# Attention steps regrouped into one TensorE visit per layer step, and the split of g moved forward, in a fused attention and feed-forward kernel

## The reference

```
q_d, k_d, v_d = means over 4 neighbouring tokens of q, k, v        # B=4, H=8, S=576, D=64
out_up    = repeat(softmax(q_d k_d^T / 8) v_d, 4)                   # coarse attention, 144 x 144
out_local = softmax(mask(q k^T / 8, |i-j| < 4)) v                   # banded attention
x = (out_up + out_local) as [2304 tokens, 512]
x = max(0.01 h, h) @ w_out    with h = x @ w_in                     # layer 1, d_ff = 2048
x = (h - tanh(h)) @ w_out2    with h = x @ w_in2                    # layer 2
```

## Time and profile before

| | |
|---|---|
| median of 3 runs | 996.45 us (994.6 to 997.91) |
| profiled execution, its own time | 992.21 us |
| span of the profiled execution | 990.4 us |
| outside the span | 1.8 us |
| PE busy | 955.1 us, 96% |
| weight load on PE busy | 891.5 us, 90% |
| DVE, ACT, POOL busy | 583.2, 554.5, 410.9 us (59%, 56%, 41%) |
| mean granted TensorE clock | 0.991 |
| layer 1, from its first hidden group to its last down group | about 67.8 to 580.4 us |

### The profile page before, as it was taken

How to read it: one execution, slowest core, us unless ns; L and a number is a source line. 1 busy time by engine, 2 the same in 40 slices (tenths; PEclk the granted TensorE clock), 3 DMA queues, 4 the chain that set the end, 5 groups by cost and what they waited for, 6 DMA issues and landing times.

```text
span 990.4 us, 19687 instructions
## 1 busy us (share of the span) xinstructions
PE 955.1 (96%) x6960; PEld 891.5 (90%) x6960; DVE 583.2 (59%) x1066; ACT 554.5 (56%) x1355; POOL 410.9 (41%) x341
## 2 busy tenths in 40 slices
PE   6788999999999999999999999999999999999998
PEld 5678999999999999999999999889899899898996
DVE  5556653663555546536324867876676676766764
ACT  3445544544645536445354767775575666766654
POOL 3446631823625517327071747633233233233232
PEclk9979999999999999999999999999999999999999
DMA  5762421122012201210200302100000000000000
GB/s 125 163 180 64 129 50 26 25 49 49 23 26 49 49 22 26 49 27 1 65 1 23 117 13 85 43 34 0 1 32 1 32 0 0 32 0 0 32 1 32
DMA packets 87222, 41.48 MB, mean 42 GB/s; under 512 B 59777, under 2 KB 80769, under 8 KB 87169
## 3 DMA queue, kind: packets, MB, share of 16 engines
q1 hardware_dynamic: 87168, 40.78, 15.4%
HBM read 36.04 MB, written 4.72 MB: 41 GB/s over the span
## 4 chain that ended last, share of the span: by engine, by line
PE 76%; POOL 6%; ACT 6%; DVE 5%; issue 3%; DMA 2%; SPq 2%; ACTq 0%; POOLq 0%; DVEq 0%
PE ph L473 11%; PE ph L475 11%; PE ph L474 11%; PE acc L549 6%; PE acc L550 6%; PE acc L551 6%; PE acc L502 6%; PE acc L503 5%; PE acc L504 5%; PE banks L371 2%; PE banks L403 2%; DVE g_lo L871 2%; POOL pl L992 2%; PE banks L390 2%; POOL g_lo L1038 1%
## 5 line engine op out<-in xcount | busy, mean ns | idle before, releaser
L1038 POOL TENSOR_TENSOR g_lo<-scratch,g_hi 128x384 fp32r<-128x384 f32 x96 | 125.6, 1309 | 257.7 <-ACT g_hi L663 257.7
L886 DVE TENSOR_TENSOR g<-g,ph 128x288 f32<-128x288 f32 x128 | 57.9, 453 | 187.7 <-ACT g L683 186.8
L1008 POOL TENSOR_TENSOR in_lo<-w_whole,in_hi 128x512 fp32r<-128x512 f32 x64 | 84.0, 1312 | 160.8 <-ACT in_hi L647 159.4
L473 PE MATMUL ph<-x_hi,w_hi_a 128*128 128x288 f32 (+1 forms) x448 | 144.5, 322 | 1.9 <-DVE x_lo L866 1.9
L475 PE MATMUL ph<-x_hi,w_lo_a 128*128 128x288 f32 (+1 forms) x448 | 140.4, 313 | 0.0
L474 PE MATMUL ph<-x_lo,w_hi_a 128*128 128x288 f32 (+1 forms) x448 | 140.3, 313 | 0.0
L683 ACT ACTIVATE g<-ph 128x288 f32<-128x288 f32 x128 | 52.5, 410 | 155.9 <-PE ph L475 154.4
L922 DVE SCALAR_TENSOR_TENSOR scratch<-scratch,ph 128x384 f32<-128x384 f32 x96 | 53.2, 554 | 108.4 <-ACT scratch L728 103.8
L1013 POOL TENSOR_TENSOR out_lo<-w_whole,out_hi 128x512 fp32r<-128x512 f32 x64 | 86.5, 1351 | 56.2 <-ACT out_hi L651 55.6
L727 ACT ACTIVATE scratch<-ph 128x384 f32<-128x384 f32 x96 | 46.8, 488 | 108.4 <-PE ph L475 106.8
L871 DVE TENSOR_TENSOR g_lo<-g,g_hi 128x288 fp32r<-128x288 f32 x128 | 90.5, 707 | 2.7 <-ACT g_hi L663 2.7
(11 more groups left out here) (162 smaller groups left out, 2689.9 us busy)
## 6 DMA issues: line engine op xcount, KB each, us to landing
out_dram<-o_stage SPq DMA_DIRECT2D x18, 256.0 KB, 2.0
w_whole<-in_moe_w_in_dram SPq DMA_DIRECT2D x16, 256.0 KB, 4.2
w_whole<-in_moe_w_out_dram SPq DMA_DIRECT2D x16, 256.0 KB, 4.3
qn<-in_q_dram SPq DMA_DIRECT2D x28, 144.0 KB
kn<-in_k_dram SPq DMA_DIRECT2D x28, 144.0 KB
v4n<-in_v_dram SPq DMA_DIRECT2D x28, 144.0 KB
vw<-in_v_dram SPq DMA_DIRECT2D x28, 122.5 KB
scratch<-in_moe_w_in_dram SPq DMA_DIRECT2D x8, 256.0 KB, 2.7
```

The lines of the kernel that those rows point to most:

```text
L473: pe.matmul(bank, whi, x_hi[:, c, 0:width], start=(c == 0), stop=False)
L1008: pool.tensor_tensor(in_lo[:, f % 2, :], w_whole[:, f - KEPT, 0:DM], in_hi[:, f % 2, :].bitcast(F32), ALU.subtract).then_inc(in_lo_done, 1)
L1038: pool.tensor_tensor(g2_lo[:, f % 3, :], g2[:, f % 2, :], g2_hi[:, f % 3, :].bitcast(F32), ALU.subtract).then_inc(g_lo_done, 1)
```

## The change

The 17 attention steps of a later pair are cut into 8 groups, one per step f of layer 1, and 16 groups (two pairs) fill the 16 steps of a mixed tile. A group's PE part is issued as one visit, behind the down group. Steps (8, 9, 10) have no PE part. The first two groups of the next pair stand in the last two steps of a tile, as steps 0 to 3 did before.

The chain leak, max, rounding, rest is now done for step f within step f on ACT and DVE, ahead of their attention steps; before, rounding and rest of step f-1 came behind leak and max of step f. The max writes back into the PSUM tile `ph1`, the rounding and the rest read it there, and H(f+2), which overwrites it, waits for the rest (`g_lo_done`) and no longer for the max. `split_in` stands ahead of the rounding, `split_out` of step f at the end of step f on ACT and POOL; before, it was at the start of step f+1 (for the last one behind `next_x` on ACT).

```diff
+GROUPS = ((0, 1), (2, 3), (4, 5), (6, 7), (8, 9, 10), (11, 12), (13, 14), (15, 16))
+GROUP_HEAD = 2
-        def later(slot, tile):
-            return (slot + HEAD) % STEPS, A, 2 * tile + 2 + (slot + HEAD) // STEPS
+        def later(f, tile, last):
+            if f < last:
+                pair, group = divmod(f + GROUP_HEAD, len(GROUPS))
+                for step in GROUPS[group]:
+                    yield step, A, 2 * tile + 2 + pair
...
 # PE
-                wait_from(pe, g_done, n - 1)
+                wait_from(pe, g_lo_done, n - 1)
...
                     if f < CF and not (begun and f == 0):
                         hidden1(tile, f)
-                    between(2 * f)
                     if ahead and f == CF + LAG1 - 1:
                         hidden1(tile + 1, 0)
                     if f >= LAG1:
                         down1(tile, f - LAG1)
-                    between(2 * f + 1)
+                    for step, s, i in later(f, tile, last):
+                        attention(step, s, i)
...
 # ACT
-                    if f - 1 >= KEPT:
-                        split_out(tile, f - 1)
                     if f < CF:
                         act.wait_ge(h_done, n + 1)
-                        wait_from(act, g_lo_done, n - 1)
+                        wait_from(act, g_done, n - 1)
                         act.activation(g1[:, f % 2, :], ph1[:, f % 2, 0:T1], ACT.Copy, scale=0.01)\
                             .then_inc(leak_done, 1)
                     if f == 0:
                         keep_before()
-                    if f:
-                        split_g(n - 1, f - 1, g1[:, (f - 1) % 2, :], g1_hi)
-                    between(2 * f)
                     if KEPT <= f + 2 < CF:
                         split_in(tile, f + 2)
+                    if f < CF:
+                        split_g(n, f, ph1[:, f % 2, 0:T1], g1_hi)
+                    for step, s, i in later(f, tile, last):
+                        attention(step, s, i)
                     extra(f)
-                    between(2 * f + 1)
+                    if KEPT <= f < CF:
+                        split_out(tile, f)
...
 # DVE
-                dve.tensor_tensor(g1_lo[:, f % 3, :], g1[:, f % 2, :], g1_hi[:, f % 3, :].bitcast(F32),
+                dve.tensor_tensor(g1_lo[:, f % 3, :], ph1[:, f % 2, 0:T1], g1_hi[:, f % 3, :].bitcast(F32),
...
-                        dve.tensor_tensor(g1[:, f % 2, :], g1[:, f % 2, :], ph1[:, f % 2, 0:T1], ALU.max)\
+                        dve.tensor_tensor(ph1[:, f % 2, 0:T1], g1[:, f % 2, :], ph1[:, f % 2, 0:T1], ALU.max)\
                             .then_inc(g_done, 1)
                     if f == 0:
                         keep_before()
-                    if f:
-                        lo_of_g1(n - 1, f - 1)
-                    between(2 * f)
+                    if f < CF:
+                        lo_of_g1(n, f)
+                    for step, s, i in later(f, tile, last):
+                        attention(step, s, i, (i + 2) // CD, (i + 2) % CD)
                     extra(f)
-                    between(2 * f + 1)
...
 # POOL
-                    if f - 1 >= KEPT:
-                        split_out(tile, f - 1)
-                    between(2 * f)
                     if KEPT <= f + 2 < CF:
                         split_in(tile, f + 2)
-                    between(2 * f + 1)
+                    for step, s, i in later(f, tile, last):
+                        attention(step, s, i)
+                    if KEPT <= f:
+                        split_out(tile, f)
```

More of the change, by code:

```diff
@@ L505, in down1, with layer1 @@
                 last.then_inc(y_done, 1)
-            def layer1(tile, between, begun=True, ahead=True):
+            def layer1(tile, last, begun=True, ahead=True):
                 for f in range(CF + LAG1):
@@ L561, in layer2 @@
                         down2(tile, f - LAG2)
[L563 to L570, removed]
             pe.wait_ge(const_ready, 1)
@@ L576, in _ @@
             pe.wait_ge(B.bank_free[1], uses1(2, 0))
-            mixed(0, begun=False)
+            layer1(0, CF, begun=False)
             with pe.Fori(1, MIXED - 1) as tile:
-                mixed(tile)
-            mixed(MIXED - 1, 2 * STEPS - HEAD)
+                layer1(tile, CF)
+            layer1(MIXED - 1, CF - GROUP_HEAD)
             for tile in range(MIXED, TILES1):
-                layer1(tile, nothing, ahead=tile < TILES1 - 1)
+                layer1(tile, 0, ahead=tile < TILES1 - 1)
             layer2(0, begun=False)
@@ L669, in keep_y, with layer1 @@
                         .then_inc(y_kept_act, 1)
-            def layer1(tile, between, extra, keep_before, ahead):
+            def layer1(tile, last, extra, keep_before, ahead):
                 for f in range(CF + 1):
@@ L698, in next_x, with mixed @@
                 split_x(x1_hi, T1, tile, CF * tile)
[L700 to L704, removed]
+            def mixed(tile, keep_before, last=CF):
+                layer1(tile, last, nothing, keep_before, lambda: next_x(tile + 1))
             def nothing(f=None):
@@ L779, in _ @@
                 mixed(tile, lambda: keep_y(tile - 1))
-            mixed(MIXED - 1, lambda: keep_y(MIXED - 2), 2 * STEPS - HEAD)
+            mixed(MIXED - 1, lambda: keep_y(MIXED - 2), CF - GROUP_HEAD)
             for tile in range(MIXED, TILES1):
                 last = tile == TILES1 - 1
-                layer1(tile, nothing, w2a if last else nothing, lambda: keep_y(tile - 1),
+                layer1(tile, 0, w2a if last else nothing, lambda: keep_y(tile - 1),
                        nothing if last else lambda: next_x(tile + 1))
@@ L1014, in split_out, with layer1 @@
                                    ALU.subtract).then_inc(out_lo_done, 1)
-            def layer1(tile, between):
-                for f in range(CF + 1):
+            def layer1(tile, last):
+                for f in range(CF):
                     if isinstance(tile, int) and tile == 0 and EARLY <= f + 2 < KEPT:
                         split_kept(f + 2)
-                    if f - 1 >= KEPT:
-                        split_out(tile, f - 1)
-                    between(2 * f)
                     if KEPT <= f + 2 < CF:
                         split_in(tile, f + 2)
-                    between(2 * f + 1)
[L1027 to L1034, removed]
+                    for step, s, i in later(f, tile, last):
+                        attention(step, s, i)
+                    if KEPT <= f:
+                        split_out(tile, f)
             def lo_of_g2(tile, f):
@@ L1077, in _ @@
                 attention(step, s, i)
-            mixed(0)
+            layer1(0, CF)
             with pool.Fori(1, MIXED - 1) as tile:
-                mixed(tile)
-            mixed(MIXED - 1, 2 * STEPS - HEAD)
+                layer1(tile, CF)
+            layer1(MIXED - 1, CF - GROUP_HEAD)
             with pool.Fori(MIXED, TILES1) as tile:
-                layer1(tile, nothing)
+                layer1(tile, 0)
             for f in range(CF):
```

## The result

The changed kernel takes 1013.37 us (median of 4 runs, 1012.1 to 1014.97), the kernel before 996.7 us (4 runs): ratio 1.0175, 95% interval 1.0158 to 1.0191. I had forecast 1004 us with a range up to 1011. The direction was right, and the size was less than half of what came. The profiled execution took 1015.0 us, its span is 1013.2 us.

A forecast was written before the change was run, and what follows sets the result against it. PE, busy 96% of the span, was taken to bound the kernel; the terms summed to +7.7 us on the profiled 992.2 us, and the same sum on the median of 996.45 gave 1004 us, range 997 to 1011.

The forecast's parts named there:

- The bound and the places: PE's order of work sets the time; in mixed tiles it stops at the turn and the ahead-run hidden group.
- The first pair's chain: Softmax chain of a tile's first pair: waiting for the same step's rounding twice delays the turn 1.2 us, +6.1 us total.
- The rest in PSUM: On DVE, the rest reading PSUM escapes POOL's hold: mean near 0.45 us, no stop for `g_lo`.
- The first `x_lo`: At a mixed tile's start, POOL's `out_lo` holds it: a 1.45 us stop in place of 0.46, +5.0 us for five.
- The first tile: PE's 2.59 us wait for the rest, held by POOL's weight split, goes; with joined visits -1.5 us.
- The second pair: In each tile's second pair, a chain of 11.0 us and a stop of 0.6 in place of 0.4, +1.2 us for six.
- rival C: POOL's queue in the second pair decides, DVE is held and D(10) waits for `out_lo`: another 7.8 us, 1012 us; chance 0.10.
- rival A: At tile starts `x_lo` slips ahead of `out_lo` or ACT finishes sooner; the seven starts cost nothing: 997.4 us; chance 0.10.
- rival B: Softmax chain less stiff, row maximum starting before 214.4; neither pairs nor starts stall: -8.7 us, 988 us; chance 0.12.
- The start of a tile: `out_lo` on POOL holds the first `x_lo`: +5.0 us for five mixed starts, +1.8 us for two plain ones.
- The joined visits: Attention visits on PE joined, fewer returns to large matmuls: 0.36 us saved a pair, -3.9 us total.
- The plain starts: At the two plain tiles' starts, `out_lo` holds `x_lo` and PE waits: +0.9 us each, +1.8 us total.

The follow-up runs named there:

- e3: Changed kernel with the grouping alone: leak, max, rounding and rest as before the change, g in SBUF; 1017.34 us, ratio 1.022.
- e4: Kernel before with the forward chain alone: rounding and rest of a step in that step, max and rest in PSUM; 1001.79 us, ratio 1.006.
- e5: Changed kernel with VectorE's row maximum and row sum ahead of the rest of the same step; 998.95 us, ratio 1.003.
- e2: Changed kernel with POOL's three sums of v of a tile's first pair moved behind that pair's normalizations; 1002.68 us, ratio 1.0073.
- e6: Changed kernel with the last step's out_hi behind x_hi on ScalarE, and row maximum and row sum ahead of the rest on VectorE; 985.59 us, ratio 0.9898.
- e1: Changed kernel with the last step's out_hi behind the next tile's four x_hi on ScalarE, as before the change; 997.84 us, ratio 1.002.

## Why the forecast fell short

**Right.** The bound and the places: PE stops at the turn and at a tile's start, and nowhere else in the mixed tiles. The first pair's chain: 1.2 forecast, 1.14 measured, undone by e3, made alone by e4, and taken away by e5. The rest in PSUM is free of POOL: 458 ns on average where it was 667. The first `x_lo` is held by `out_lo`: a stop of 1.45 forecast, 1.40 measured. The first tile: -1.5 and -1.9. The second pair: a chain of 11.0 us forecast, 10.95 measured (250.48 to 261.43), and a stop of 0.6 forecast, 0.55 measured. No queue on POOL decides there (rival C); what I had not seen is that this pair's subtraction on DVE lay under `out_lo` before (1.83 us) and is free of it now (0.82 us), since `out_lo` stands later. Nothing slipped in ahead of `out_lo` (rival A), and rival B's condition did not hold: the row maximum started 3.6 us after the scores ended, where it was 3.1.

**The step that failed** is "The start of a tile". It says that POOL starts `out_lo`, that this holds the first `x_lo`, and goes on as if POOL were idle after it. The three sums of v of the next pair, which stand right behind that `out_lo` in POOL's queue, have no term and no sentence in it. They could be seen in the trace of the kernel before, whose `out_lo` ended at 207.23:

```profile
207.40 0.74 POOL L985 TENSOR_TENSOR vd<-v4n 72x256 f32<-72x256 f32 x1 [0.17 <-DMA vw<-in_v_dram]
```

There the four `x_lo` were long done (204.51 to 206.07). Now the three sums alternate with the other `x_lo`: 1.5 us a start, 7.5 us (shown by e2). They also made a pattern of short stops behind a long one, behind which TensorE ran at half clock at three starts: 4.4 us, in no term and no rival of mine. Both together are 11.9 us; the two sums in the table lie 11.6 apart, and the forecast and the median 9.4.

**Mis-sized terms.** The joined visits saved about 0.9 us a tile, not 0.7, nearly all of it behind the products with v. The plain starts cost 1.36 us each, not 0.9; 0.25 of that is a late H(2), whose PSUM tile now waits for the rest behind `keep_y`. In layer 2 one more down group waits for POOL than before (0.95 us), where POOL splits that layer's weights (a stop that e4 has too and e3 has not, so it comes with the forward chain; why, no run shows), and the little won at the end of layer 1 is given back.

**Open**: why the clock falls at three starts of the changed kernel and at one of e5, with the same stops. What PE does between the starts does not tell them apart: in e5 the tiles ahead of all of the last four starts take 68.22 to 68.23 us with the same stops, and only the last one falls; in the changed kernel the tiles ahead of the second start (it holds) and the third (it falls) take 70.34 and 70.35 us. The moment at which the stops come may count. No run here moves it alone.

## What to carry to other kernels

When an instruction moves, write down the whole queue of the engine behind it and let each entry start as early as its own waits allow: what follows at once may now meet work of another engine that was long done before. When a producer is made earlier by waiting on another engine in the middle of a queue, put the work that the critical chain needs ahead of that wait. Here that was worth 12.3 us (e6 against e1); with `out_hi` behind `x_hi` as well, a loss of 1.7% became a gain of 1.0%, and with the next tile's x further ahead one of 1.3%. And a stop of PE is to be priced with what the clock may do behind it.

## What the hardware showed

A VectorE instruction with two SBUF inputs and a GpSimd instruction that reads SBUF alternated strictly, one for one, four times in a row: 3.89 us for the four VectorE instructions, which take 1.56 us where GpSimd is idle, while POOL's three sums, 0.74 us elsewhere, took up to 0.94. The granted clock fell to 0.50 within a row of stops in which PE was still shown 76% busy, stayed there for about 3.4 us and cost about 1.5 us of PE's time each time; PE was busy throughout at half clock before it rose. A single stop of 1.4 us (1.13 to 1.23 us of idle time) left it at 1.00 in all five starts of the one traced execution of e2. With the same four stops it fell at four starts of ten, in the changed kernel and e5 together.
